# Attention, experts and FFN in one kernel: normalising moved to VectorE, copies to ScalarE, logits into attention

## What is computed

```python
scores = np.where(mask, scale * q @ k.T + bias, -1e9)          # window of 128, causal
attn = np.exp(scores - max(scores))
attn = attn / (sum(attn) + 1e-9)
x = attn @ v                                                    # 2304 x 512
logits = x @ w_gate                                             # 2304 x 8
P = np.exp(logits - logits.max())
for _ in range(8):
    P /= P.sum(1, keepdims=True) + 1e-9
    P /= P.sum(0, keepdims=True) + 1e-9
    P *= N / E
out = sum(P[:, e:e + 1] * (np.maximum(x @ w1[e], 0.0) @ w2[e]) for e in range(8))
h = out @ w_in                                                  # d_ff 2048
result = np.maximum(0.01 * h, h) @ w_out
```

## Time and profile before

| what | us |
| --- | --- |
| three timed runs | 2203.27, 2211.54, 2211.78 (median 2211.54) |
| the profiled execution | 2200.45 |
| its span, first to last instruction | 2198.7 |
| TensorE busy | 2084.9 (95%) |
| VectorE busy | 1159.6 (53%) |
| ScalarE busy | 621.4 (28%) |
| GpSimd busy | 1214.7 (55%) |
| mean granted TensorE clock | 0.971 |

### The profile page before, as it was taken

The page is one execution under the profiler, slowest core; times in us unless marked ns, Lnnn a source line. Parts: engine busy times, 40 slices in busy tenths (PEclk is TensorE's granted clock), DMA queues, the critical chain, the costliest instruction groups (busy, mean ns, idle before and its releaser), DMA issues.

```text
span 2198.7 us, 35718 instructions
## 1 busy us (share of the span) xinstructions
PE 2084.9 (95%) x12475; PEld 1855.0 (84%) x12475; DVE 1159.6 (53%) x2552; ACT 621.4 (28%) x1712; POOL 1214.7 (55%) x935
## 2 busy tenths in 40 slices
PE   4766998999999999999999999999999999999999
PEld 3544887899999999998899999999999998998998
DVE  3443256665555555555545545545545555666565
ACT  3454121222222222223322222222222233334332
POOL 7788344445545556546645555555555556567551
PEclk7898699999999999999999999999999999999999
DMA  2221010111111111111111111111111101111211
GB/s 99 74 83 62 20 39 31 43 43 43 47 44 40 47 46 39 47 47 39 49 48 39 48 48 38 48 48 38 48 47 39 45 32 58 39 39 49 92 39 44
DMA packets 30868, 104.72 MB, mean 48 GB/s; under 512 B 3920, under 2 KB 3920, under 8 KB 30800
## 3 DMA queue, kind: packets, MB, share of 16 engines
q1 hardware_dynamic: 30800, 103.84, 13.8%
HBM read 99.11 MB, written 4.72 MB: 47 GB/s over the span
## 4 chain that ended last, share of the span: by engine, by line
PE 86%; POOL 8%; DVE 3%; issue 2%; DMA 0%; ACT 0%; SPq 0%; DVEq 0%; POOLq 0%
PE bank L1156 15%; PE bank L1157 15%; PE bank L1158 14%; PE bank L1131 13%; PE bank L1136 13%; PE bank L1134 13%; POOL sc L345 5%; POOL x_lo L447 1%; PE bank L1045 1%; PE bank L1114 1%; POOL up_lo L361 1%; DVE sc L721 1%; DVE row_sum L820 1%; DVE pt_sb L738 1%; PE bank L1172 0%
## 5 line engine op out<-in xcount | busy, mean ns | idle before, releaser
L1131 PE MATMUL bank<-x_hi,up_hi 128*128 128x256 f32 (+1 forms) x2240 | 670.8, 299 | 21.9 <-ACT u L555 13.4
L811 DVE SCALAR_TENSOR_TENSOR acc<-bank,gate,acc 128x512 f32<-128x512 f32 x495 | 371.6, 751 | 575.2 <-PE bank L1158 575.2
L1136 PE MATMUL bank<-x_hi,up_lo 128*128 128x256 f32 (+1 forms) x2240 | 670.9, 300 | 0.0
L1134 PE MATMUL bank<-x_lo,up_hi 128*128 128x256 f32 (+1 forms) x2240 | 670.2, 299 | 0.0
L1156 PE MATMUL bank<-down_hi,hs_hi 128*128 128x512 f32 x1440 | 571.1, 397 | 0.4 <-DVE hs_lo L923 0.4
L1157 PE MATMUL bank<-down_lo,hs_hi 128*128 128x512 f32 x1440 | 570.7, 396 | 0.0
L1158 PE MATMUL bank<-down_hi,hs_lo 128*128 128x512 f32 x1440 | 563.0, 391 | 0.0
L1131 PEld LDWEIGHTS bank<-x_hi,up_hi 128*128 128x128 f32 x2240 | 427.9, 191 | 50.9 <-ACT u L555 14.3
L1134 PEld LDWEIGHTS bank<-x_lo,up_hi 128*128 128x128 f32 x2240 | 428.0, 191 | 23.6
L1136 PEld LDWEIGHTS bank<-x_hi,up_lo 128*128 128x128 f32 x2240 | 428.2, 191 | 0.1
L361 POOL TENSOR_TENSOR up_lo<-stage_up,up_hi 128x1792 fp32r<-128x1792 f32 x80 | 324.7, 4058 | 6.4
(11 more groups left out here) (108 smaller groups left out, 1901.2 us busy)
## 6 DMA issues: line engine op xcount, KB each, us to landing
stage_up<-w_up SPq DMA_DIRECT2D x80, 512.0 KB, 3.2
stage_down<-w_down SPq DMA_DIRECT2D x80, 512.0 KB, 3.2
qk<-qk SPq DMA_DIRECT2D x16, 608.0 KB, 3.7
v_nat<-v SPq DMA_DIRECT2D x16, 320.0 KB, 2.9
result<-acc SPq DMA_DIRECT2D x16, 256.0 KB, 2.6
result<-acc SPq DMA_DIRECT2D x4, 128.0 KB, 2.8
wg<-moe_w_gate SPq DMA_DIRECT2D x1, 16.0 KB, 5.5
```

Source lines behind the costliest of these rows:

```text
L811: last = d.scalar_tensor_tensor(out=to, in0=y[:, :], scalar=share(g, tile, e), in1=to, op0=ALU.mult, op1=ALU.add)
L1131: m.matmul(to[:, 0:n], up_hi[s][:, w], x_hi[u][:, x], start=first and c == 0, stop=False, skip_group_check=True)
L1134: m.matmul(to[:, 0:n], up_hi[s][:, w], x_lo[u][:, x], start=False, stop=False, skip_group_check=True)
L1136: last = m.matmul(to[:, 0:n], up_lo[s][:, w], x_hi[u][:, x], start=False, stop=c == 1, skip_group_check=True)
```

## The change

- GpSimd's `normalise` and VectorE's `invert` become one `normalise` on VectorE: add, invert, scale.
- VectorE's two copies go to ScalarE: group 1's probabilities (`copy_pt` with group 1, ahead of the next step's group 1 exponentials) and `copy_out` (behind the exponentials of group 2).
- GpSimd's `first_operand` is gone. The sums for unit 0 are made on VectorE and the casts on ScalarE in the last attention step, the low parts on GpSimd (four) and VectorE (three, `first_lows(0)`). The seven low parts for unit 1 are all VectorE's, at the end of unit 0 (`first_lows(1)`).
- Logits of the first three batches are computed inside attention, one call of four (in every fourth step eight) matmuls a step; those of the last batch stand as blocks of four between the products of unit 0. They have a PSUM bank of their own now, and the maximum is taken one unit earlier.
- The Sinkhorn steps stand at unit ends: `columns_to_share` and the next `rows_to_one`, one after the other, behind the last output tile of units 3 to 11.
- `up_lo` is made in seven instructions of 256 columns instead of one of 1792, `down_lo` in four of 256 instead of one of 1024.
- At the later turns GpSimd makes four low parts and VectorE three (the last one behind `sum_11` of the next unit).
- ScalarE copies the third product (`copy_u2`) ahead of its wait for `sum_11`.
- TensorE's attention steps are written out instead of looped.

```diff
-            def normalise(i, g_, s):
...
-                pool.wait_ge(exp_done, GROUPS * i + g_ + 1)
-                g.tensor_scalar(esum_eps[0:rows, st], esum[0:rows, st], EPS, None, ALU.add).then_inc(eps_added, 1)
...
+            def normalise(i, g, s):
...
+                dve.wait_ge(exp_done, GROUPS * i + g + 1)
+                d.tensor_scalar_add(esum_eps[0:rows, st], esum[0:rows, st], EPS).then_inc(eps_added, 1)
...
+                for _, _, _, nk, _, c, st in segments(g, s):
+                    part = sc[0:rows, c:c + nk]
+                    last = d.tensor_scalar(part, part, einv[0:rows, st:st + 1], None, ALU.mult)
...
-                g.tensor_tensor(up_lo[s][:, :], stage_up[:, FG:], up_hi[s][:, :], ALU.subtract).then_inc(up_split, 1)
+                for op in range(OPS):
+                    part = slice(op * FG, (op + 1) * FG)
+                    last = g.tensor_tensor(up_lo[s][:, part], raw(op), up_hi[s][:, part], ALU.subtract)
+                last.then_inc(up_split, 1)
...
             def step(i, s, first=False, last=False):
+                if not first:
+                    copy_pt(i - 1, 1, 1 - s)
                 exponentials(i, 1, s)
                 if not first:
                     copy_pt(i - 1, 2, 1 - s)
                 copy_pt(i, 0, s)
                 exponentials(i, 2, s)
+                if not first:
+                    copy_out(i - 1)
...
+            casts(0, -1, 0)
+            copy_pt(ITERS - 1, 1, 1)
+            casts(0, -1, 1)
+            copy_pt(ITERS - 1, 2, 1)
+            casts(0, -1, 2)
+            copy_out(ITERS - 1)
+            casts(0, -1, 3)
...
                 casts(phase, k, 0)
+                copy_u2(k, u)
                 act.wait_ge(c11_done, k + 1)
                 a.activation(hs_hi[u][:, hidden_part(u, 0, 0)], b_b[:, 0:n], ACT.Relu).then_inc(hi_done, 1)
-                copy_u2(k, u)
...
-                if 4 <= k < 4 + ROUNDS:
-                    if point == 0:
-                        if k == 4:
-                            dve.wait_ge(gate_exp, 1)
-                        rows_to_one(k - 4)
-                    if point == 3:
+                if 3 <= k < 4 + ROUNDS and point == 3:
+                    if k == 3:
+                        dve.wait_ge(gate_exp, 1)
+                    else:
                         columns_to_share(k - 4)
+                    if k < 3 + ROUNDS:
+                        rows_to_one(k - 3)
...
                 values(i, 0, s, first)
+                if i >= KD:
+                    logits(i // KD - 1, i % KD)
+                    if i % KD == KD - 1:
+                        logits(i // KD - 1, KD)
                 transpose_p(2, s)
```

More of the change, by code:

```diff
@@ L667, in _ @@
             unit(0, 0, phase=0)
[L668 removed]
+            for k in range(1, 3):
                 unit(k, k % 2)
@@ L1074, in values, with logits @@
                     last.then_inc(pv_done, 1)
+            def logits(b, n):
+                tile, _, t, rows, p0 = [(tile, *part) for tile in range(TILES) for part in token_parts(tile)
+                                        if part[0] == b % 2][n]
+                c = logits_at(b // 2 * TILES + tile)
+                for kd in range(KD):
+                    x = b * HALF + kd * S + t
+                    last = m.matmul(b_tail[p0:p0 + rows, c:c + E], x_raw[:, x:x + rows],
+                                    wg[:, kd * E:(kd + 1) * E], start=kd == 0, stop=kd == KD - 1)
+                return last
             def step(i, s, first=False, last=False):
```

385 lines of the change are left out of this document (163 added, 222 removed).

## The result

| | before | after |
| --- | --- | --- |
| timed runs, median | 2211.66 us (2203.27 to 2212.34, 4 runs) | 2063.31 us (2061.92 to 2064.29, 4 runs) |
| profiled execution | 2200.45 | 2064.29 |
| its span | 2198.7 | 2062.5 |
| mean granted clock | 0.971 | 0.994 |

The ratio is 0.9337, with a 95% interval of 0.9314 to 0.9360. Between the spans lie 136.2 us; the profiled execution of before lay 11 us under its own median and that of after 1 us above, which is the rest of the 148 us between the medians.

The account below looks back on a forecast made before the run. GpSimd's scaling with its hand-offs to VectorE was taken to bound attention, TensorE everything from 410.1 us. Terms 55 + 4 + 12 + 22 + 21 + 6.5 = 120.5 us off 2200.45 gave 2080, plus 5: 2085 us, range 2060 to 2125.

Parts of the forecast that it names:

- (a): Attention steps: each falls from 12.35 to 8.4 us, 55 us won over 14 steps, 4 more in the last.
- VectorE's share: Attention steps: VectorE busy 6.5 us a step after the change, 8.9 if scaling runs at twice the price.
- (b): First attention step: falls from 25.3 to 13.3 us, 12 won, bounds 6 and 16.
- (c): Units 0 and 1: 18 and 16 us, 34 together instead of 56.2, 22 won, bounds 28 and 50.
- (d): Sinkhorn units 2 to 10: 108 us instead of 128.9, 21 won, bounds 10 and 22.7.
- (e): Two units at the later turns: 6.5 us won of 9.6, bounds 3 and 9.6.
- (f): GpSimd's weight splits in pieces: 1.7 us more a granule on GpSimd, hidden behind TensorE.
- The offset: Timed runs against profiled execution: runs lie 3 to 11 us above it, so 5 us were added.
- steps of 10.4 us from in-order waits: Rival in attention: in-order waits on three engines cost 30 us more, 2115 us; chance 0.15.
- a low clock in attention: Rival in attention: TensorE at 1.2 GHz throughout makes the kernel slower, 2222 to 2232 us; chance 0.03.
- a scaling that gets no turn between pieces: Rival: Sinkhorn units keep 128.9 us and step 0 stays near 25, 2116 us; chance 0.05.
- The third, the drain: Rival at attention's end: late operands and low parts make units 0 and 1 take 50 us, 2101; chance 0.12.

Follow-up runs that it names:

- e1: Changed kernel with the normalising (addition and scaling) back on GpSimd, copies still on ScalarE and logits in attention; 2140.95 us, ratio 0.9699.
- e7: Kernel before with the normalising alone moved to VectorE, copies left on VectorE, operands and logits as before; 2151.30 us, ratio 0.9745.
- e6: Changed kernel with all 80 logit matmuls in unit 0, as blocks between its products, none in attention; 2080.27 us, ratio 0.9424.
- e12: e11 with GpSimd's first split of weights started when step 5 of attention is scaled, not at 15 us; 2058.47 us, ratio 0.9322.
- e10: Changed kernel with 16 of unit 0's 20 logits moved into attention, reading the third batch's tokens, for timing alone; 2069.34 us, ratio 0.9376.
- e11: Changed kernel with GpSimd making four of VectorE's seven unit 1 low parts, and two unit 1 sums behind unit 0's sums of products; 2060.66 us, ratio 0.9328.
- e4: Changed kernel with the small scaling back ahead of `sum_11` and `copy_u2` behind its wait, pieces kept; 2068.20 us, ratio 0.9355.
- e8: Kernel before with only the low parts of the weights cut into pieces of 256 columns; 2192.23 us, ratio 0.9934.
- e3: Changed kernel with GpSimd's two low parts of the weights whole again, Sinkhorn steps left at unit ends; 2073.02 us, ratio 0.9376.
- e5: Changed kernel with all three Sinkhorn edits undone: whole low parts, scaling ahead of `sum_11`, `copy_u2` behind its wait; 2090.17 us, ratio 0.9454.
- e2: Changed kernel with the copies of group 1's transposes and of the output back on VectorE, normalising kept there; 2087.87 us, ratio 0.9455.

## Why the prediction held, and where it did not

The forecast was 2085 us in a range of 2060 to 2125, faster with 0.95. It came out at 2063.31, inside the range near its low end, and every term that missed by more than 1 us missed on the same side.

- **The bound of before**, GpSimd's scaling and its hand-offs, was right: e1 puts it back and 64.5 us of idle transposes return; e7 takes it alone and 39 us go in steps 1 to 14.
- **(a) The steps.** I said 8.4 us, near the largest sum of 8.1, and gave 0.3 for in-order waits. From step 2 on they take 7.90; with step 1 at 10.9 us the fourteen intervals are 113.6 us, 59.3 won for 55, and the last step 5.1 for 4. Three sizes in it were off: TensorE's share, ScalarE's, and the waits. The 7.34 busy us of TensorE are not one step's: the stretch of 11.7 us takes in three matmuls of the next step, 77 for 74. Step 1 of the kernel before by itself:

```profile
39.40:50.66 11.26, 7.00 (x74) 5.11 (x74) 5.58 (x30) 5.99 (x24) 8.79 (x13) 1.00 0.30 102
```

  That agrees with the 7.06 of e6 (91.83 / 13), where no logits are in it. With them TensorE is busy 7.81 us in a step of the changed kernel (steps 2 to 14), so four logits take it 0.75, much as I had said (0.8 for five), but they lengthen the step by 0.37 alone, since without them ScalarE is the bound. ScalarE's sum, said to be 8.0, is 7.3 in e6 (95.01 / 13). And in-order waits, said to be 0.3, are the 0.1 between 7.81 and 7.90.
- **VectorE's share** was right in size: 6.63 us in the step shown where I said 6.5, 371 ns for one scaling beside GpSimd's 923.
- **(b) Step 0.** 12 won was said, 15.7 measured: step 0 takes 11.7 us, not 13.3, and begins 2 us earlier. Near the upper bound of 16; e12 shows that VectorE beside the split still held 3.3 us of step 0.
- **(c) Units 0 and 1.** 34 said, 29.1 measured. I started unit 0 at half clock, because the drain of before was at 0.73; the shorter drain runs at 1.00, and unit 0 began at full clock. The seven low parts on VectorE took 1.31 to 1.65 us each beside GpSimd's pieces, which I had given as up to 1.56, and they do hold TensorE up, 2.57 us. The low clock of 10.2 us stays with 4 of the 20 logits (e10) and goes when TensorE's wait goes (e11).
- **(d) Sinkhorn.** 108 said, 108.4 measured, 20.5 won for 21. That a piece ends the wait was right (e4, e8). That the scaling never takes over 1 us was not: the longest took 1245 ns. And the second half of the reason, the place at the unit's end, adds only 2.1 us once the pieces are there (e4).
- **(e) Turns.** 6.5 said, 7.6 measured in units 129 and 145, and the next wait is the one named, for the split. The waits of TensorE from 1679 to 1693 us:

```profile
PE bank L1089 <- POOL up_lo L350: 0.7, 1, 0.7
```

  Unit 65 is a further turn, which I had not counted: 11.68 us for 12.69, 1.0 more. That VectorE now makes the fifth low part is what won here: e3 and e5, with the low parts of the weights whole as before, take 11.7 and 12.2 us in these units for 16.6.
- **(f) The pieces are hidden**: right in the steady units (1774.59 of 1780.10 us of TensorE busy), not in the turns, where the split is awaited: 1.7 us in all, by e3.
- **The offset.** By the terms the sum came out 136.2 for 120.5. The other 6 of the 22 us between 2085 and 2063 are the offset: I added 5 for the runs of before lying above their profiled execution, and those of after lie 1 us under theirs.

Of the rivals, steps of 10.4 us from in-order waits did not come, nor a low clock in attention (0.97), nor a scaling that gets no turn between pieces. The third, the drain, came in part: low parts of operands do hold unit 0 up, but against a shorter start. e7, though, shows a step in which VectorE does stretch, once the copies stay with it.

What the row showed of the clock was 0.64 in units 0 and 1 with TensorE busy. My row was right for the kernel before and did not carry over: with 20 of the 80 logits left in units 0 and 1, in blocks of four in unit 0, the 37.5 us at 1.2 GHz became 10.2, and none in e11 and e12. That it went with the logits is what e6 and e7 show; that it went with nothing else is not shown.

The Trainium skill ("TensorE: Matmul & The Clock Gate", section "What's actually happening") has activity release the throttle. In e11 and e12 unit 0 ran in 9.4 us without a gap, all at 2.4 GHz, and the trace agrees with the rule. In unit 0 of e6 TensorE was busy 35.06 of 36.70 us, and the clock was 1.2 GHz for 29.6 of them; there the trace does not agree, and the measurement decides.

## What to carry to other kernels

When an engine is named as the bound of a pipelined step, add up the busy time of every engine per step as it would be after the move: the engine with the largest sum was busy 93 to 98% of the new step each time (VectorE in e7 and e2, ScalarE in e6, TensorE in the changed kernel), and the second move was worth its 1.1 us only because the first had made VectorE the bound. A long GpSimd instruction held up the short VectorE additions and scalings in SBUF that met it, so cut it into pieces or move it to where the others have slack; but cut only where nobody waits for its end. Small matmuls that must be done somewhere were cheapest here a few at a time in the attention steps (0.09 us each in most, more in the steps with eight). Between the products they brought the clock down, sixteen in a row (e6) as well as one by one (before, e7).
